# Channel attention folded into a feed-forward layer, fp32 on one core: VectorE forms the summed weight factors, token loads move to pair 0, the weight ring comes in three requests

## The reference

```python
# q, k, v: (2, 6016, 256), tau: scalar, w_in: (256, 2048), w_out: (2048, 256)
qn = q / (norm(q, axis=1) + 1e-6);  kn = k / (norm(k, axis=1) + 1e-6)
a  = softmax(kn.transpose(0, 2, 1) @ qn / tau, axis=-1)   # (2, 256, 256), channel attention
x  = (v @ a).reshape(12032, 256)
h  = x @ w_in
out = (h * sigmoid(h)) @ w_out                            # (12032, 256)
```

## Time and profile before

| what | value |
|---|---|
| median of three runs | 1072.94 us |
| the profiled execution: its own time | 1070.89 us |
| its span, first to last instruction | 1069.1 us |
| mean granted TensorE clock | 0.995 |
| busy share: PE / DVE / ACT / POOL | 97% / 87% / 84% / 28% |
| chain that ended last, by engine | PE 71%, DVE 6%, ACT 3%, issue 3%, DMA 2% |
| DMA | 197 MB, mean 184 GB/s |

### The profile page before, as it was taken

One profiled execution on the slowest core, in us unless ns is written; L12 is line 12 of the kernel. 1 busy time (PEld: TensorE's weight loads), 2 busy tenths in 40 slices (PEclk: granted clock), 3 DMA queues, 4 the chain that ended last, 5 costly groups with the idle time before them and its releaser, 6 DMA issues.

```text
span 1069.1 us, 15160 instructions
## 1 busy us (share of the span) xinstructions
PE 1034.2 (97%) x4584; PEld 851.6 (80%) x4584; DVE 934.1 (87%) x1307; ACT 898.7 (84%) x1580; POOL 297.6 (28%) x323
## 2 busy tenths in 40 slices
PE   9999998989999999999978999999999999999997
PEld 8987776767888888888867777888888888888886
DVE  6887685689889899899899999899899899899898
ACT  7997676778898998898867788898898898988875
POOL 3695231143120121221273662121121211210100
PEclk9999999999999999999999999999999999999999
DMA  9993421397786885876975885885876876975742
GB/s 358 397 366 89 151 92 66 133 265 176 199 194 152 215 196 135 216 176 148 255 150 143 225 193 124 219 188 132 235 173 152 217 173 147 229 168 130 176 134 88
DMA packets 107921, 197.06 MB, mean 184 GB/s; under 512 B 9424, under 2 KB 42448, under 8 KB 107712
## 3 DMA queue, kind: packets, MB, share of 16 engines
q1 hardware_dynamic: 82720, 150.07, 43.2%
q0 software_dynamic: 24544, 45.17, 25.9%
q10 hardware_dynamic: 576, 0.85, 0.2%
HBM read 145.82 MB, written 50.23 MB: 183 GB/s over the span
## 4 chain that ended last, share of the span: by engine, by line
PE 71%; DVE 6%; ACT 3%; issue 3%; DMA 2%; SPq 1%; DVEq 0%; POOL 0%; ACTq 0%; POOLq 0%
PE ps_h L823 12%; PE ps_h L825 12%; PE ps_h L824 12%; PE ps_o L883 6%; PE ps_o L884 6%; PE ps_o L885 6%; PE ps_h L883 5%; PE ps_h L885 5%; PE ps_h L884 5%; DVE t_raw L1584 1%; DVE g_lo L1572 1%; DMA ring<-s_dram 1%; PE ps_o L870 1%; PE ps_o L872 1%; PE ps_o L874 1%
## 5 line engine op out<-in xcount | busy, mean ns | idle before, releaser
L1572 DVE TENSOR_TENSOR g_lo<-h,g_hi 128x512 fp32r<-128x512 f32 (+1 forms) x296 | 205.4, 696 | 24.5 <-ACT g_hi L1206 23.2
L1206 ACT ACTIVATE g_hi<-h 128x512 fp32r<-128x512 f32 (+1 forms) x296 | 182.5, 620 | 10.2 <-PE ps_h L885 3.8
L648 POOL DMA_DIRECT2D out_t_dram<-fl_sb x70 | 61.6, 879 | 437.0 <-ACT fl_sb L1234 428.8
L823 PE MATMUL ps_h<-b_hi,a_hi_mid 128*128 128x512 f32 (+1 forms) x336 | 132.7, 395 | 6.1 <-ACT h L1183 3.1
L825 PE MATMUL ps_h<-b_hi,a_lo_mid 128*128 128x512 f32 (+1 forms) x336 | 130.9, 390 | 0.0
L824 PE MATMUL ps_h<-b_lo,a_hi_mid 128*128 128x512 f32 (+1 forms) x336 | 130.7, 389 | 0.0
L1558 DVE TENSOR_TENSOR h<-ps_h,w 128x512 f32<-128x512 f32 (+1 forms) x96 | 65.2, 679 | 61.5 <-PE ps_h L825 41.7
L883 PE MATMUL ps_h<-g_hi,ring 128*128 128x512 f32 (+1 forms) x264 | 103.7, 393 | 13.5 <-DVE g_lo L1572 7.2
L1606 DVE TENSOR_TENSOR gx_lo<-t_raw,gx_hi 128x1024 fp32r<-128x1024 f32 (+1 forms) x88 | 107.8, 1225 | 0.6 <-ACT gx_hi L1213 0.6
L1584 DVE TENSOR_TENSOR t_raw<-h 128x1024 f32<-128x1024 f32 (+1 forms) x88 | 107.4, 1221 | 0.0
L883 PE MATMUL ps_o<-gx_hi,ring 128*128 128x512 f32 (+1 forms) x264 | 102.2, 387 | 0.7 <-DVE gx_lo L1616 0.4
(11 more groups left out here) (217 smaller groups left out, 2772.7 us busy)
## 6 DMA issues: line engine op xcount, KB each, us to landing
ring<-s_dram SPq DMA_DIRECT2D x88, 640.0 KB, 5.0
ring<-s_dram SPq DMA_DIRECT2D x88, 256.0 KB, 3.1
out_t_dram<-fl_sb POOLq DMA_DIRECT2D x72, 256.0 KB, 6.2
x_raw<-v_t_dram SPq DMA_DIRECT2D x58, 256.0 KB, 4.4
x_raw<-v_t_dram POOLq DMA_DIRECT2D x45, 256.0 KB, 7.1
out_t_dram<-o_sb SPq DMA_DIRECT2D x27, 256.0 KB, 4.5
out_t_dram<-o_sb POOLq DMA_DIRECT2D x27, 256.0 KB, 6.0
qk<-q_dram SPq DMA_DIRECT2D x17, 384.0 KB, 11.0
```

What stands on the lines that cost most here:

```text
L823: nc.tensor.matmul(out, w_hi, x_hi, start=start, stop=False, skip_group_check=True)
L1206: nc.scalar.activation(g_hi[:, g, 0:tok], h[:, g, 0:tok], ACT.Copy).then_inc(hi[g], 1)
L1572: nc.vector.tensor_tensor(g_lo[:, g, 0:tok], h[:, g, 0:tok], g_hi[:, g, 0:tok].bitcast(F32), ALU.subtract).then_inc(lo[g], 1)
```

## The change

- **Factors of w_out.** Four groups of two pairs instead of eight parts. DVE forms the sums of a group in four instructions of 128x256 (`sum_group`), ACT rounds all four formed blocks in one of 128x1024 (`round_group`), DVE splits in one (`split_group`); all within step 0 and the first period of step 1. F2, F4 and F1 are stored straight from `wo_hi` and `wo_lo` (`store_plain`). POOL's `part` is gone.
- **Second batch.** DVE forms the sums for all pairs in four instructions of 128x1024 in step 0 (`sum_a1`); `a1_dram` holds seven blocks a pair. In steps 5 and 6 SP loads 448 KB a pair into `a_lo`, ACT rounds in one instruction of 128x896 (`round_a1`), DVE splits in one. POOL's `prepare_a1` is gone.
- **Token loads.** `load_x` is five blocks, for the next step, at pair 0, behind `begin_c12` and a ring request on SP; the sixth (`load_x_base`) follows the split of T4. POOL's adds: two at pair 0, one each at pairs 1, 2 and 5. T4 is rounded at pair 7 and split at pair 0 of the next step.
- **Ring.** Three requests a pair: F1, F3; F2, F4 (waits for `p6_done`); F7, F5, F6.
- **Ends.** In the opening, `probs_hi` has a buffer for each batch, `round_probs(1)` comes three instructions earlier on ACT and `split_probs(1)` ahead of `sum_a(0, 1)` on DVE. Pair 95's second product is done plainly with eight products, without T sums. Step 0's results leave from buffers of their own instead of `x_raw`.

```diff
 SP
             def load_x(step):
                 places = ((X_T3, 0, 1), (X_B11, 0, 0), (X_B21, 1, 0), (X_B22, 1, 1))
                 if step:
-                    places += ((X_T1, 0, 0), (X_T2, 0, 0))
+                    places += ((X_T1, 0, 0),)
...
+            def load_x_base(step):
+                load_x_block(step, X_T2, 0, 0).then_inc(v_base, 16)
...
+            def load_ring_c(n):
+                sp.wait_ge(p6_done, n + 1)
+                load_ring(n, F2, F1, ring_c)
...
             def load_a1(pair):
-                sp.wait_ge(a_split, PAIRS)
-                if pair >= 2:
-                    sp.wait_ge(a1_split, pair - 1)
-                sp.dma_start(a1_raw[pair % 2][:], a1_dram[:, pair]).then_inc(a1_loaded[pair % 2], 16)
+                sp.wait_ge(a1_raw_saved, 32)
+                sp.wait_ge(a1_sums_saved, 32)
+                sp.wait_ge(p4_done, SWITCH + pair + 1)
+                sp.dma_start(a_lo(pair).bitcast(F32), a1_dram[:, pair]).then_inc(a1_loaded[pair % 2], 16)
...
             for n in range(FIRST + 2, PERIODS):
                 it, pair = divmod(n, PAIRS)
+                if n in a1_load_at:
+                    load_a1(a1_load_at[n])
                 load_ring_a(n)
...
                 if it > 1 and pair == 0:
                     begin_c12(it - 1)
...
+                load_ring_c(n)
+                if pair == 0 and it + 1 < ALL:
+                    sp.wait_ge(x_split, x_groups(it) - 1)
+                    load_x(it + 1)
                 load_ring_b(n)
-                if n + 1 in reload_at:
-                    load_a1(reload_at[n + 1])
-                if pair == PAIRS - 1 and it + 2 < ALL:
-                    sp.wait_ge(x_split, x_groups(it + 1))
-                    load_x(it + 2)
+                if pair == 0 and it + 1 < ALL:
+                    sp.wait_ge(x_split, x_groups(it))
+                    load_x_base(it + 1)
 POOL
             def add_x_first(step):
-                pool.wait_ge(v_loaded, 96 * step + 64)
-                add_x(step, X_T2, 0, 1).then_inc(t_first, 16)
+                pool.wait_ge(v_loaded, 80 * step + 64)
                 add_x(step, X_T1, 0, 1).then_inc(t_first, 16)
                 add_x(step, X_T3, 1, 1).then_inc(t_first, 16)
             def add_x_second(step):
-                pool.wait_ge(t_first, 48 * step)
+                pool.wait_ge(v_base, 16 * step)
+                add_x(step, X_T2, 0, 1).then_inc(t_second, 16)
+            def add_x_third(step):
+                pool.wait_ge(t_second, 32 * step - 16)
                 add_x(step, X_T2, 1, 1).then_inc(t_second, 16)
...
             for n in range(FIRST + 2, PERIODS):
                 it, pair = divmod(n, PAIRS)
                 if n - 2 <= PAIRS * FINAL - 1:
                     add_flushed(n - 2)
...
-                if pair == (0 if it > 1 else 2) and it + 1 < ALL:
+                if it > 1 and pair == 0 and it + 1 < ALL:
                     add_x_first(it + 1)
-                if pair == (1 if it > 1 else 3) and it + 1 < ALL:
+                if it > 1 and pair == 1 and it + 1 < ALL:
                     add_x_second(it + 1)
-                if pair == (5 if it > 1 else 6) and it + 1 < ALL:
+                if pair == 2 and it + 1 < ALL:
                     add_x_third(it + 1)
-                if n == FIRST + 4:
-                    part(7)
-                if n in reload_at:
-                    prepare_a1(reload_at[n])
+                if pair == 5 and it + 1 < ALL:
+                    add_x_fourth(it + 1)
 ACT and DVE
+            GROUP_ROUND_AT = {2: 0, 4: 1, 6: 2, 7: 3}
+            ROUND_X_FIRST = {4: 0, 5: 1, 6: 2, 7: 3}
+            ROUND_X = {2: (B11,), 3: (T2, B21), 4: (T1,), 5: (B22,), 6: (T3,), 7: (T4,)}
+            ROUND_X_SEVENTH = {2: (B11,), 3: (T2,), 4: (T1,), 6: (B21, B22), 7: (T3, T4)}
+            SPLIT_X = {3: (B11,), 4: (T2,), 5: (B21,), 6: (T1,), 7: (B22, T3)}
+            SPLIT_X_SEVENTH = {4: (B11, T2), 6: (T1,), 7: (B21, B22, T3)}
+        A1_ROUND_AT = (42, 44, 45, 46, 47, 50, 52, 53)
+        A1_SPLIT_AT = (44, 46, 48, 49, 50, 51, 53, 54)
...
 DVE, first_step (step 0, period n)
-                if 1 <= n < PAIRS - EARLY - 1:
+                if 1 <= n < PAIRS - 1:
                     split_a(0, n + 1)
+                if n == 1:
+                    sum_a1(0)
+                if n == 2:
+                    sum_group(0)
+                if n == 3:
+                    split_group(0)
+                    sum_a1(3)
+                if n == 4:
+                    sum_group(1)
+                if n == 5:
+                    split_group(1)
+                if n == 6:
+                    sum_group(2)
+                if n == 7:
+                    split_group(2)
+                    sum_group(3)
                 make_c22(n, TOK)
...
+                if n == 1:
+                    sum_a1(1)
+                if n == 2:
+                    sum_a1(2)
+                if n == 5:
+                    split_x(1, T1, T2)
+                if n == 6:
+                    split_x(1, B11, B22)
+                if n == 7:
+                    split_x(1, T3, T3)
...
-                if PAIRS - EARLY - 1 <= n < PAIRS - 1:
-                    split_a(0, n + 1)
...
-                if n in PARTS_AT:
-                    split_part(PARTS_AT[n])
-                if n in SPLIT_X_FIRST:
-                    split_x(1, *SPLIT_X_FIRST[n])
 TensorE, the end
-            def closing_products(n):
-                f_t1(n - 1)
-                f22(n)
-                f_t2(n - 1)
-                f11(n)
-                f_t1(n)
-                f_t2(n)
-                f_t3(n)
-                pe.wait_ge(fl_added, PAIRS - 2)
-                f21(n)
-                f_t4(n)
+            def closing_products():
+                f_t1(LAST - 1)
+                f_t2(LAST - 1)
...
+                last_pair(F1, H11, m1, False)
+                last_pair(A21_RING, H11, m4, False)
...
+                last_pair(F2, H22, m3, False)
...
+                last_pair(F1, H12, m3, False).then_inc(last_summed, 1)
...
+                last_pair(F2, H21, m1, False).then_inc(last_summed, 1)
+                last_pair(F4, H21, m4, False).then_inc(last_summed, 1)
+                pe.wait_ge(last_nv, 1)
+                last_pair(F4, H22, m5, True)
+                last_pair(A21_RING, H12, m5, False).then_inc(last_summed, 1)
```

More of the change, by code:

```diff
@@ L127, in channel_attention_ffn @@
             wp_raw += [sb("wp_raw1", [P, PAIRS, 4, P], stack=early)]
+        with ExitStack() as early:
+            stages = [sb(f"stage{n}", [P, 2, 2, 4, P], stack=early) for n in range(2)]
         t13_raw = sb("t13_raw", [P, 2, TOK])
@@ L149, in channel_attention_ffn @@
             w_in_lo = sb("w_in_lo", [P, CK, F], F32R, stack=early)
-            probs_hi = sb("probs_hi", [P, CK, C], F32R, stack=early)
+            probs_hi = [sb(f"probs_hi{b}", [P, CK, C], F32R, stack=early) for b in range(B)]
             probs_lo = sb("probs_lo", [P, CK, C], F32R, stack=early)
@@ L163, in channel_attention_ffn @@
         with ExitStack() as early:
-            parts = [sb(f"parts{n}", [P, 2 * FACTORS, P], stack=early) for n in range(2)]
+            first_stage = sb("first_stage", [P, 2, 2, 4, P], stack=early)
         a_hi_last = sb("a_hi_last", [P, EARLY, FACTORS, P], F32R)
         a_lo_last = sb("a_lo_last", [P, EARLY, FACTORS, P], F32R)
+        with ExitStack() as early:
+            a1_sums = sb("a1_sums", [P, PAIRS, 3, P], stack=early)
         b_hi += [sb("b_hi1", [P, FACTORS, TOK], F32R)]
@@ L391, in load_chunk, with load_x_block @@
                     sp.dma_start(qk[s][:, 1, 0:rows, :], rows_of(k, g)).then_inc(slot_loaded[s], 16)
+            def load_x_block(step, place, c, t):
+                first, n = tokens_of(step)
+                return sp.dma_start(x_raw[:, place, 0:n], v_t[step // STEPS, c * P:(c + 1) * P,
+                                                              first + t * n:first + (t + 1) * n])
             def load_x(step):
@@ new lines, in load_group, with store_group @@
+            def load_group(j):
+                blocks = w_out[4 * j * P:4 * (j + 1) * P, :].rearrange("(a f p) c -> p a f c", a=2, f=2)
+                for place, (f, c) in enumerate(((1, 0), (0, 1), (1, 1), (0, 0))):
+                    sp.dma_start(stage_of(j)[1][:, :, place, :], blocks[:, :, f, c * P:(c + 1) * P]).then_inc(
+                        group_loaded[j % 2], 16)
+            def store_group(j):
+                sp.wait_ge(group_split, j + 1)
+                for half in range(2):
+                    sp.dma_start(s_dram[2 * j:2 * j + 2, :, half, F3:].rearrange("a p f m -> p a f m"),
+                                 stage_of(j)[half]).then_inc(group_stored, 16)
@@ L1363, in pair_step @@
                     copy_m5(it - 1)
+                if n == LAST:
+                    copy_last_m1()
                 if it < FINAL:
-                    for block_ in (ROUND_X if it > 1 else ROUND_X_SECOND).get(pair, ()):
```

(15 more changed lines are left out.)

443 lines of the change are left out of this document (237 added, 206 removed).

## The result

The changed kernel takes 1101.19 us in the median of four runs (1096.53 to 1104.04), the kernel before beside it 1074.68 (1072.3 to 1076.77): a ratio of 1.0241, interval 1.0204 to 1.0277. It is slower, by 26.5 us where the forecast had no change, and above the range's upper end of 1092. The profiled execution took 1102.01 us with a span of 1100.2; TensorE's mean granted clock is 0.976 (0.995 before).

What follows compares the result with a forecast made beforehand. TensorE was taken as the bound, with 38.5 us lost where weights are prepared. 1070.9 - 31.8 of gains + 33 for token loads = 1072.1, or 1074 on the median's scale; own range 1062 to 1084, overall 1046 to 1092.

Steps and rivals of the forecast that it cites:

- What bounds it, and where the change hurts: TensorE bounds most steps; the token loads at pair 0 are the largest single term, a cost of 33 us.
- Token loads at pair 0: Steps 2 to 10: POOL's load wait delays pair 1's flush DMA; 3.5 us per wide step, 5 in step 5, sum 33.
- as third in a row I take 7.7: Assumed landing time in us of pair 1's flush DMA, issued behind two adds, putting it 4.1 us after ACT wants it.
- Half a us in hand: TensorE's assumed slack behind the late flush of pair 1, leaving 3.5 us lost in each wide step.
- First rival: Pair 1's flush DMA lands after 5.1 us, TensorE loses 9 us in all: 1050, down to 1041; chance 0.30.
- half of all flush DMAs: Argument for the flush landing in time: this share was said to be as fast as 5.1 us.
- Second rival: T2's adds, each waiting for the one before, delay ACT's rounding in pair 3: 18 us, 1092; chance 0.20 for above 1084.
- Steps 5 and 6: Second batch's preparation taken from POOL: gains 12.3 and 4.2 us, bounds together 9 to 21; ACT fits barely, at 69.1.
- Step 0 and opening: Gain 4.4 us in step 0 from POOL's removed preparation (bounds 1 and 7.9), 1.0 in the opening from earlier rounding.
- Step 1: The 3.6 us wait for token loads behind output stores goes: gain 7.1 us with step 2, bounds 4 and 9.
- End: Closing stretch done plainly, 30 matmuls and one addition: gain 2.8 us, bounds 1 and 3.4.
- Ring: Three requests a pair move the same bytes with one more issue on an idling queue: no effect on time.
- the same 8.6: Assumed us from the token loads' issue on SP at 440.43 to POOL getting them at 449.0.

Runs made afterwards that it cites:

- thin ones: The changed kernel with the two x adds (T1, T3) ahead of pair 1's flush DMA cut from 512 to 32 token columns: 1073.77 us.
- the two-request ring alone: The changed kernel with the token loads moved ahead of begin_c12 on SP, and the ring back from three requests a pair to two: 1049.74 us.
- early loads alone: The changed kernel with the five token loads on SP moved ahead of begin_c12 and the second ring request in pair 0: 1046.88 us.
- the fastest kernel: The changed kernel with token loads ahead of begin_c12, own buffer for (0,0), group 1's loads before stores, x adds behind pair 1's flush, POOL's adds spread: 1032.03 us.

## Why the prediction was wrong, point by point

- **What bounds it, and where the change hurts: right.** The largest cost was named as the flush DMA of pair 1 behind POOL's wait for the token loads. It was forecast to leave 14.7 us after the seed; it leaves at 13.9 to 15.3.
- **The failed step: "Token loads at pair 0", its sum of 33 us.** It is 62, by three terms. The landing, "as third in a row I take 7.7", is 7.3 to 9.5 with a median of 8.7. "Half a us in hand" isn't there: the flush lands 5.1 us too late on average (after 18.3 us, or 17.0 in step 5), and the seed of pair 2 is late by 5.2. These two turn 33 into 47. And the granted clock after each stall, 15 us, has no term at all, although the kernel before shows a dip too. The forecast's own upper end, 1084, took a landing of 8.7 but the same half us and no clock, so 43 stood for what cost 62.
- **First rival, "the flush lands in time": wrong here, right in mechanism.** It needed 5.1 us. A flush DMA alone does land in 4.4 in the median in the changed kernel (pairs 4 to 7), but not with two whole adds ahead; thin ones gave 5.8. Nor were "half of all flush DMAs" as fast as 5.1 before: 23 of 80 were. The estimate of 2.6 us by the Trainium skill's page "DMA: Bandwidth & Descriptors" (Anatomy of one DMA — SWDGE) is met by no accumulating DMA of 256 KB in any run, where the shortest landing is 3.8; those of 16 KB took 2.3 to 5.3. A plain one of 256 KB from POOL, the first flush of step 1, did land in 2.3 us in the changed kernel.
- **Second rival, T2's chain: didn't decide.** The wait shows with the two-request ring alone, up to 2.3 us. In the changed kernel T2's adds took 4.1 to 5.9 us each, not the 8.2 to 9.9 of the sum.
- **Steps 5 and 6: right.** 12.3 and 4.2 forecast; with the stall out of the way 12.8 and 5.0 (71.4 and 78.2), 9.9 and 5.0 with early loads alone. ACT fits, with more room than forecast: 67.0 us busy in step 5 of the fastest kernel, not 69.1. The cause was told too simply: leaving out POOL's sums alone gave 6.1 of the 15 to 18 us. The rest came with the whole rebuilding (POOL's roundings gone, one load and one split a pair, other periods) and isn't shown part by part.
- **Step 0 and opening: right in sum, by luck.** 5.4 forecast, 5.3 measured: the opening gave more (the first seed 2.9 sooner, cause not looked into), step 0 less. The load of group 1 was late by 2.56, not 0.7, and the clock was at half for 3.4 us soon after.
- **Step 1: wrong term.** 7.1 forecast, 2.8 measured. The wait of 3.6 went, and one of 3.15 came that I hadn't looked for: `fl` as output buffer. With a buffer of its own step 1 is 78.0, 7.1 less than before.
- **End: right.** 2.8 forecast, 2.3 measured.
- **Ring: right in time, at nothing**, not in its working: it shortens the landings on the other queue.
- **Two small readings, without effect.** The way of the loads is 8.4 us (431.57 to 439.94), and was carried over as "the same 8.6"; and 0.55 us between POOL's issues, which is what the changed trace shows (0.54), doesn't follow from the 2.67 and 0.86 named for it.

## What to carry to other kernels

On an in-order issuing engine a wait is paid by whatever stands behind it: place each wait behind the issue that something else is counting on, and spread accumulating DMAs so that none that is waited for has whole ones right ahead of it. Price a stall on the chain of TensorE with what the clock takes after it, here a third on top. And when an experiment removes a stall only in part, look for the next member of the same chain: pair 1's and pair 2's flush had to be freed both before the gain of 4% came out.
